# Moving one SBUF tile ahead of four others in the order of allocation

## The reference

```python
# convolution: 8 heads of 24 channels, 7 taps, softmax over the taps of a head
x_unf = x_pad[:, idx, :].reshape(B, S, K, H, group)
out = np.einsum('hk,bskhg->bshg', softmax(weight), x_unf)
# first MLP, d_ff = 1536
x = (sigmoid(x @ w_gate) * (x @ w_val)) @ w_out
# second MLP, d_ff = 2048
r = np.maximum(x @ w_in, 0.0)
x = (r * r) @ w_out
```

## Time and profile before

| | |
|---|---|
| median of three runs | 2481.82 us |
| profiled execution | 2481.82 us |
| its span, first to last instruction | 2480.1 us |
| mean granted TensorE clock | 0.996 of 2.4 GHz |
| TensorE matmul busy | 2371.3 us, 96% |
| TensorE weight load busy | 1955.1 us, 79% |
| VectorE busy | 1838.8 us, 74% |
| ScalarE busy | 1154.0 us, 47% |
| GpSimd busy | 133.2 us, 5% |

### The profile page before, as it was taken

How to read it: one execution, slowest core, us unless ns; L and a number is a source line. 1 busy time by engine, 2 the same in 40 slices (tenths; PEclk the granted TensorE clock), 3 DMA queues, 4 the chain that set the end, 5 groups by cost and what they waited for, 6 DMA issues and landing times.

```text
span 2480.1 us, 54540 instructions
## 1 busy us (share of the span) xinstructions
PE 2371.3 (96%) x20868; PEld 1955.1 (79%) x20868; DVE 1838.8 (74%) x3556; ACT 1154.0 (47%) x2332; POOL 133.2 (5%) x140
## 2 busy tenths in 40 slices
PE   5899999999999999999999999999999999999997
PEld 4788877877778777778777787777787777877886
DVE  8777777777777777777777777777777777777654
ACT  3444444444444444444444444444444444444444
POOL 0000000000000000000000000000000000000000
PEclk9999999999999999999999999999999999999998
DMA  4211111101111111111111111111111111111101
GB/s 111 73 30 39 44 47 27 47 21 45 46 30 44 32 36 44 47 30 44 25 43 44 31 43 35 32 44 47 30 44 27 40 44 33 41 38 30 39 25 30
DMA packets 98846, 99.40 MB, mean 40 GB/s; under 512 B 7680, under 2 KB 84992, under 8 KB 98816
## 3 DMA queue, kind: packets, MB, share of 16 engines
q1 hardware_dynamic: 98800, 98.99, 16.2%
q10 hardware_dynamic: 16, 0.00, 0.0%
HBM read 19.27 MB, written 12.58 MB: 13 GB/s over the span
## 4 chain that ended last, share of the span: by engine, by line
PE 87%; DVE 7%; issue 3%; ACT 3%; DMA 1%; SPq 0%; DVEq 0%; POOL 0%; ACTq 0%
PE hp L369 49%; PE acc L415 21%; PE acc L420 14%; DVE hid_t L674 2%; PE hp L370 2%; ACT act_t L552 2%; DVE lo L688 1%; DVE hid_t L678 1%; DVE y L722 1%; PE acc L416 1%; DVE y L731 1%; ACT act_t L555 1%; DVE xT L708 1%; PE acc L421 1%; DMA xs<-xs 0%
## 5 line engine op out<-in xcount | busy, mean ns | idle before, releaser
L369 PE MATMUL hp<-xs,w 64*128 64x512 f32 x5760 | 1416.9, 389 | 41.6 <-DMA xs<-y_rest 24.1
L370 PE MATMUL hp<-xs,w 64*128 64x512 f32 x5760 | 1417.0, 389 | 0.0
L369 PEld LDWEIGHTS hp<-xs,w 64*128 64x128 f32 x5760 | 1058.9, 185 | 266.3 <-issue 30.2
L370 PEld LDWEIGHTS hp<-xs,w 64*128 64x128 f32 x5760 | 1058.9, 185 | 2.2
L688 DVE TENSOR_TENSOR lo<-hid_t,hi 128x512 fp32r<-128x512 f32 x896 | 611.1, 682 | 0.5
L415 PE MATMUL acc<-hi,wo 64*128 64x512 f32 x1792 | 553.0, 388 | 52.2 <-DVE y L731 52.2
L678 DVE TENSOR_TENSOR hid_t<-act_t 128x512 f32<-128x512 f32 x512 | 351.4, 687 | 297.2 <-ACT act_t L555 296.5
L552 ACT ACTIVATE act_t<-hp 128x512 f32<-128x512 f32 x384 | 230.1, 599 | 711.4 <-PE hp L369 711.4
L416 PE MATMUL acc<-hi,wo 64*128 64x512 f32 x1792 | 553.0, 388 | 0.0
L555 ACT ACTIVATE act_t<-hp 128x512 f32<-128x512 f32 x512 | 307.1, 600 | 485.4 <-PE hp L370 473.4
L674 DVE TENSOR_TENSOR hid_t<-hp,act_t 128x512 f32<-128x512 f32 x384 | 264.9, 690 | 256.6 <-ACT act_t L552 253.7
(11 more groups left out here) (63 smaller groups left out, 1927.9 us busy)
## 6 DMA issues: line engine op xcount, KB each, us to landing
xs<-xs SPq DMA_DIRECT2D x160, 256.0 KB, 3.8
xs<-y_rest SPq DMA_DIRECT2D x128, 128.0 KB, 3.3
xin<-in_x_dram SPq DMA_DIRECT2D x32, 384.0 KB, 4.3
out_dram<-stage SPq DMA_DIRECT2D x32, 384.0 KB, 2.6
moved<-y_parts SPq DMA_DIRECT2D x32, 128.0 KB, 2.2
moved<-z_parts SPq DMA_DIRECT2D x64, 64.0 KB, 2.0
stage<-in_moe_w_out_dram SPq DMA_DIRECT2D x7, 384.0 KB, 3.2
stage<-in_moe_w_in_dram SPq DMA_DIRECT2D x12, 128.0 KB, 3.0
```

What stands on the lines that cost most here:

```text
L369: low = pe.matmul(hp[:, 2 * pair, :], w[lower, wk, c], xs[lower, xk, :], start=s, stop=e)
L370: up = pe.matmul(hp[:, 2 * pair + 1, :], w[upper, wk, c], xs[upper, xk, :], start=s, stop=e)
```

## The change

The declaration of `xT` moves from behind `lo` to ahead of `act_t`. Shapes, types, instructions and semaphores stay as they are.

```diff
         acc_up = sb("acc_up", [P, 2, N])
         xin = sb("xin", [P, B, D])
 
+        xT = sb("xT", [P, G, HALO + P])
         act_t = sb("act_t", [P, 2, N])
         hid_t = sb("hid_t", [P, 4, N])
         hi = sb("hi", [P, RING, N], F32R)
         lo = sb("lo", [P, RING, N], F32R)
-        xT = sb("xT", [P, G, HALO + P])
         taps = sb("taps", [P, 2, K])
         soft_w = sb("soft_w", [H, K])
         exp_w = sb("exp_w", [H, K])
```

## The result

The changed kernel takes 2513.49 us (median of 4 runs, 2512.45 to 2515.2), against 2481.81 us before: ratio 1.0128, 95% interval 1.011 to 1.0146. It is 31.7 us slower. The forecast was no change, with a range that ended at 2490 us.

A forecast was written before the change was run, and what follows sets the result against it. The prediction took TensorE's stream of 10,240 matmul pairs at 226.5 ns to bound the kernel. All its terms were 0, so the forecast stayed at 2481.8 us, with a range of 2478 to 2490 us.

The forecast's parts named there:

- What bounds the kernel: TensorE's stream of 10,240 matmul pairs at 226.5 ns each: 2319 us, nearly all of the 2439 us body.
- What moves: Only addresses: xT begins at 180352; act_t, hid_t, hi and lo 3232 bytes later, no longer on multiples of 64.
- Step 1: 4480 output pairs streaming hi or lo: 0 ns taken; bounds 26.9 us slower (6 ns a pair) and 59 us faster.
- the lower bound: 13.2 ns a pair, 59 us in all, is the most output pairs could gain, at one column per 2.4 GHz cycle.
- Step 2: VectorE and ScalarE instructions on the moved tiles: 0 taken, at most 4.6 us slower or faster.
- Steps 3 to 5: Accesses to xT, small matmuls on head_of at the start, and DMAs, which touch none of the moved tiles: 0 each.
- Rival A: Output pairs: TensorE fetches in pieces of 64 bytes or more, shifted streams touch one more; 2495.2 or 2508.7 us; chance 0.13.
- Rivals B, C and D: B: output steps 2 ns shorter, 2472.9 us (0.07); C: VectorE/ScalarE times, 2477.2 to 2486.4; D: unmoved places, 2481.8; C/D in 0.80.
- rule on runs of words: VectorE's port keeps full rate only for runs of two or more words from an 8-byte boundary; weighed, not used.

The follow-up runs named there:

- e4: The changed kernel with soft_w, exp_w and stat ahead of hi: act_t and hid_t 32 bytes off a multiple of 64, hi and lo on 128; 2480.41 us.
- e2: The changed kernel with soft_w, exp_w and stat (96 bytes) also ahead of act_t, so the four tiles start at a multiple of 128 again; 2481.68 us.
- e10: The kernel before with taps, soft_w and exp_w (128 bytes) ahead of act_t: hi and lo on a multiple of 256, weights and xs unmoved; 2515.07 us.
- e11: The kernel before with soft_w ahead of w1: every large tile 32 bytes further up, all at the same place within 256 bytes; 2484.81 us.
- e6: The kernel before with hi and lo in one common tile, beginning 16 bytes into it; 2517.40 us.
- e13: The kernel before with taps, soft_w and exp_w between wo2 and stage: weights stay, everything behind them moves to differ by 128 bytes; 2535.12 us.
- e1: The changed kernel with 32 more bytes between xT and act_t: act_t, hid_t, hi and lo start 64 off a multiple of 128; 2517.98 us.
- e14: The kernel before with hi and lo in one tile, beginning 4 bytes (one float32) into it; 2531.79 us.
- e15: The kernel before with wo1 and wo2 behind xs1: wo1, wo2, hi and lo at 32 past a multiple of 256, w1, w2 and xs at 128; 2512.76 us.

## Why the prediction was wrong

**What bounds the kernel**: right. The stream of pairs sets the time; 32.3 us of the change are in its steps, and the waits did not grow.

**What moves**: the addresses were right. The remark that every tile that TensorE streams, apart from `soft_w`, sat on a multiple of 128 was wrong for `ident` (228800, 64 past one), which the transposes stream; it holds for the 10,240 pairs. But I then asked of each operand only where it lies by itself. I never wrote down where it lies relative to the operand that TensorE reads at the same time. That `xs`, `hi`, `lo` and all weights were equal modulo 256 could be worked out from the declarations, and the change broke just that.

**Step 1, the output matmuls at 0 ns: this is the step that failed.** It measured 6.4 ns on the 4377 steps (28.2 us), against a value taken of 0 and a bound of 6 ns (26.9 us), which the range then did not reach. The value came from VectorE's taps, which pay nothing for an odd start. That was the nearest row for "a read at an odd address", but not for TensorE, which has a second read going, the weight load (184 ns of each step of 227). And there is a cost that I had no term for at all: 7.7 us on the steps of `xs`, which did not move, since the disturbance outlasts the pair that causes it. What the lower bound rests on stands: with the other engines idle at the end of the stream, the steps are as long as elsewhere, 227 ns before and 234 after.

**Step 2** (VectorE and ScalarE, 0 within 4.6 us): right. Medians of L688 and L541 moved by +2 and -1 ns, and e4 gives -0.3 us for `act_t` and `hid_t` alone. **Steps 3 to 5** (`xT`, `head_of`, DMAs at 0): right as far as e2 shows, 0.9 us with all of them moved.

**Rival A** had the engine, the main place (28.2 us on the output pairs), the sign and nearly the price: 2508.7 us at its 6 ns. Its mechanism, one more piece of a line for a stream that starts inside one, is refuted: e10 is slow on rounder addresses, e11 is fast on odd ones. I gave it 0.13, with VectorE's taps as the one argument against it, and then cut the range at 1.8 ns a pair, below its own price. The bound of 6 ns was unmeasured on the engine that sets the time, and the range should have reached it. **Rivals B, C and D** did not occur.

**The two rules of the Trainium skill.** The rule on runs of words spoke of VectorE and had no bearing on TensorE; for the long runs of the taps no start was charged (739 to 745 ns). By the 16-byte line that the page "SBUF — State Buffer" of the Trainium skill gives (section "Door 1: The DMA port swizzle"), the time would have been 2482 us. The runs differ: the changed kernel (a multiple of 16 off) costs 31.7 us, and e6, 16 bytes off, 36.7. A third statement would have misled in the same way: the page "TensorE: Matmul & The Clock Gate" of the Trainium skill, section "Step-by-step: what each phase is for", says that the streamed operand and the weight load have read ports of their own, so that loading takes nothing from the running matmul. The runs differ from that: the load's place relative to the stream is worth 54 us in e13. The measurement decides.

**What stays open.** The runs show that a weight load beside a stream at another place modulo 256 lengthens steps, by how much, and that the disturbance outlasts it. They don't show the mechanism in the memory. In e1 the output steps settle at 233.3 ns, 226.7 + 6.6, or 16 cycles at 2.4 GHz more; in e13 long stretches swing between 229 and 238. That would suit two reads that take turns at something with a period of 256 bytes and need some steps to fall into step again after a disturbance, as they do behind the waits of the kernel before; but this is only argued. Why steps that agree stay slow for one to nine steps is open too, and so is why 4 bytes cost more than 32, and whether types narrower than four bytes or full 128-row matmuls behave alike; none was run.

## What to carry to other kernels

Only this kernel was measured. In one like it, bound by a stream of matmuls, write down for every tile that TensorE reads its address modulo 256 bytes, weights and moving operands in one list, and keep them equal; a small odd-sized tile (here 3216 bytes) declared among them cost 1.3% without touching an instruction, and other disagreements cost 1.2 to 2.3%. Declare such tiles last, or pad them to a multiple of 256. And when the trace has no row for an operation on the engine that sets the time, don't let another engine's row make its price zero: keep the bound in the range.

## What the runs showed of the hardware

- Weight loads and moving operands (64 rows, float32r, 512 columns, two halves of the array side by side) that agree modulo 256 bytes step at 226.7 ns a pair; with any disagreement tried (4, 16, 32, 64, 96 and 128 bytes) nearly all steps are 224 to 241 ns, 232.8 in the mean where all disagree (e13).
- The place itself costs little: all tiles 32 bytes on cost 4.1 us (ratio 1.0007 to 1.0026), all 128 bytes on 1.9 us (0.9996 to 1.0016), of 2481.
- A disagreement is felt in the next one to nine steps (one behind the output rows of five pairs in e14, nine in the rows of eighteen projection pairs in e15), so alternating (`lo` alone, +41.5 us) can cost more than disagreeing throughout the row (`hi` and `lo`, +31.7 us).
- Where weights and moving operands agree, slow steps come only behind an interruption of the stream: in the kernel before 402 of the 1156 steps within twelve of a wait or a transpose take 229 ns or more, and 11 of the 8634 others.
- ScalarE and VectorE don't share this: `act_t` and `hid_t` 32 bytes off a multiple of 64 cost -0.3 us.
